# Output weights of the last layer: second half loaded from SyncE's queue, rounding spread over the first block, early minima, scatter waits exchanged

## What is computed

```python
# attention whose mask keeps only keys in the same hash bucket as the query
x = attn_out.transpose(0, 2, 1, 3).reshape(1536, 512)
# mixture of experts, 8 experts, each token goes to one
h = np.maximum(x[mask] @ w1[e], 0.0)
out[mask] = gate_w[mask, None] * eom[mask, e, None] * (h @ w2[e])
# last layer: 1536 x 512 -> 1536 x 2048 -> 1536 x 512
h = x @ w_in
g = np.where(h > 0.0, h, np.exp(np.minimum(h, 0.0)) - 1.0)
return (g @ w_out).astype(np.float32)
```

## Time and profile before

| | |
|---|---|
| median of 3 executions | 815.64 us (815.6 to 816.53) |
| the profiled execution, its own time | 815.6 us |
| its span, first to last instruction | 813.8 us |
| time around the span | 1.8 us |
| mean granted clock of TensorE | 0.999 |
| busy: PE, DVE, ACT, POOL | 97%, 56%, 44%, 42% |
| HBM traffic over the span | 88 GB/s |

### The profile page before, as it was taken

The page is one execution under the profiler, slowest core; times in us unless marked ns, Lnnn a source line. Parts: engine busy times, 40 slices in busy tenths (PEclk is TensorE's granted clock), DMA queues, the critical chain, the costliest instruction groups (busy, mean ns, idle before and its releaser), DMA issues.

```text
span 813.8 us, 12942 instructions
## 1 busy us (share of the span) xinstructions
PE 792.4 (97%) x4389; PEld 658.3 (81%) x4389; DVE 453.5 (56%) x801; ACT 361.6 (44%) x684; POOL 340.4 (42%) x333
## 2 busy tenths in 40 slices
PE   7999999999999889999999999999999999999996
PEld 4777777777777668888888888889889989989985
DVE  5776767777777375454454454549516415613720
ACT  4677676776677413432234330037316405602710
POOL 4334343555556049977797785044210020000000
PEclk9999999999999999999999999999999999999999
DMA  5322232111200047675567660350010020000000
GB/s 151 98 66 76 66 92 94 40 50 42 67 12 18 13 129 277 233 239 199 179 229 236 194 215 18 105 194 0 18 61 2 1 61 17 1 14 27 1 14 26
DMA packets 40942, 72.68 MB, mean 89 GB/s; under 512 B 17904, under 2 KB 24304, under 8 KB 40880
## 3 DMA queue, kind: packets, MB, share of 16 engines
q10 hardware_dynamic: 10608, 33.69, 12.7%
q1 hardware_dynamic: 26832, 26.88, 10.5%
q0 software_dynamic: 3440, 11.28, 4.3%
HBM read 60.56 MB, written 11.28 MB: 88 GB/s over the span
## 4 chain that ended last, share of the span: by engine, by line
PE 92%; DVE 4%; ACT 2%; issue 1%; POOL 1%; DMA 0%; POOLq 0%; ACTq 0%; DVEq 0%
PE pair_t L1350 16%; PE pair_s L1248 13%; PE pair_t L1263 13%; PE pair_u L1118 8%; PE bank_b L1134 8%; PE pair_s L1300 7%; PE pair_u L1300 7%; PE pair_t L1107 4%; PE pair_s L1107 4%; PE bank_b L1145 2%; PE pair_u L1227 2%; PE bank_a L1085 2%; PE bank_a L1093 1%; PE bank_a L1074 1%; DVE g_lo L1054 1%
## 5 line engine op out<-in xcount | busy, mean ns | idle before, releaser
L432 POOL TENSOR_TENSOR w_part<-w_raw,w_part 128x1024 fp32r<-128x1024 f32 x80 | 190.0, 2406 | 51.7 <-ACT w_part L654 51.0
L654 ACT ACTIVATE w_part<-w_raw 128x1024 fp32r<-128x1024 f32 x72 | 73.5, 1055 | 183.8 <-PE pair_t L1263 149.1
L1350 PE MATMUL pair_t<-w_part,g_hi 128*128 128x512 f32 x384 | 118.8, 391 | 0.0
L1248 PE MATMUL pair_s<-w_part,xs_t 128*128 x456 | 108.8, 394 | 0.4 <-DVE xs_t L932 0.4
L1263 PE MATMUL pair_t<-w_part,hid_t 128*128 x456 | 109.0, 394 | 0.0
L563 POOL DMA_INDIRECT out<-o_sb,token x12 | 11.8, 986 | 216.4 <-DVE o_sb L1026 216.4
L1248 PEld LDWEIGHTS pair_s<-w_part,xs_t 128*128 128x128 f32 x456 | 84.2, 188 | 17.8 <-issue 0.9
L1263 PEld LDWEIGHTS pair_t<-w_part,hid_t 128*128 128x128 f32 x456 | 84.4, 189 | 16.8
L1118 PEld LDWEIGHTS pair_u<-first,exps 128*128 128x128 f32 x576 | 65.2, 141 | 27.7 <-ACT exps L614 19.2
L1118 PE MATMUL pair_u<-first,exps 128*128 128x128 f32 x576 | 83.9, 277 | 3.3 <-ACT exps_t L623 1.8
L1350 PEld LDWEIGHTS pair_t<-w_part,g_hi 128*128 128x128 f32 x384 | 71.7, 188 | 14.4
(11 more groups left out here) (196 smaller groups left out, 1214.7 us busy)
## 6 DMA issues: line engine op xcount, KB each, us to landing
w_raw<-in_moe_w ACTq DMA_DIRECT2D x48, 512.0 KB, 6.5
w_raw<-in_moe_w SPq DMA_DIRECT2D x16, 512.0 KB, 8.2
ys_sorted<-ys SPq DMA_DIRECT2D x19, 256.5 KB, 5.7
w_raw<-in_moe_w_in ACTq DMA_DIRECT2D x8, 512.0 KB, 7.1
w_raw<-in_moe_w_out ACTq DMA_DIRECT2D x8, 512.0 KB, 6.6
raw<-in_q SPq DMA_DIRECT2D x16, 192.0 KB, 2.4
raw<-in_k SPq DMA_DIRECT2D x16, 192.0 KB, 2.7
v_nat<-in_v SPq DMA_DIRECT2D x16, 192.0 KB, 2.5
```

Source lines behind the costliest of these rows:

```text
L432: pool.tensor_tensor(chunk_of(w_part, n, 1, c), w_raw[n % 2][c][:, :], chunk_of(w_part, n, 0, c).bitcast(F32), ALU.subtract).then_inc(s_wl ...
L654: act.activation(chunk_of(w_part, n, 0, c), w_raw[n % 2][c][:, :], ACT.Copy).then_inc(s_whi, 1)
L1248: mm = pe.matmul(pair_s[:, h, :], xs_t[:, xp, c * P:(c + 1) * P], w_part[:, bass.ds(par, 1), wp, a:a + 512], start=c == 0 and xp == 0 and ...
L1350: mm = pe.matmul(pair_t[:, t % 2, :], gp[:, f, j * P:(j + 1) * P], w_out_p[:, wp, f, :], start=f == 0 and m == 0, stop=f == FT - 1 and m == 2)
```

## The change

1. Memory: `elu` is placed ahead of `g_lo`, so that it no longer lies over `hid_t`, but over the slots' inputs `xs_raw`.
2. SyncE: before it waits to store the last slot's `ys`, it waits for the end of the last `layer2` and issues the loads of chunks 4 to 7 of w_out.
3. ScalarE: its list of set 9 has only the four loads of the first half. The wait for the last `layer2`, four `w_hi` and four loads in front of the last layer are gone. In block 0 `w_hi` of chunk f // 2 follows every odd step f, from 1 to 15.
4. VectorE: `copy_y(18)` moves from in front of step 0 to in front of step 2 of block 0. The rest of the edit of that loop leaves its order as it was.
5. GpSimd: a scatter waits first for s_o and then for s_tok.

```diff
@@ -240,8 +240,8 @@
             sb("rows_first", [P, BT, YW])
             sb("turned_first", [P, 2, CD, NB], F32R)
             g_hi = sb("g_hi", [P, FT, NB], F32R)
+            elu = sb("elu", [P, 3, NB])
             g_lo = sb("g_lo", [P, FT, NB], F32R)
-            elu = sb("elu", [P, 3, NB])
             o_sb = sb("o_sb", [P, DM])
         w_part = keep("w_part", [P, 2, 2, SET], F32R)
 
@@ -419,6 +419,10 @@
 
 
             for n in range(SLOTS):
+                if n == SLOTS - 1:
+                    wait_release(sp, E + 1, NC1, None)
+                    for c in range(NC1, NCH):
+                        sp.dma_start(chunk_dst(E + 1, c), chunk_source(E + 1, c)).then_inc(s_wld[c], 16)
                 sp.wait_ge(s_y, n + 1)
                 sp.dma_start(ys_dram[n * P:(n + 1) * P, :], ys[:, n % 2, :]).then_inc(s_yst[n % 2], 16)
 
@@ -558,8 +562,8 @@
                                         bass.IndirectOffsetOnAxis(row_at[:, t:t + 1], 0)).then_inc(s_yg[t % BT], 16)
 
             def scatter(t):
+                pool.wait_ge(s_o, t + 1)
                 pool.wait_ge(s_tok, t + 1)
-                pool.wait_ge(s_o, t + 1)
                 pool.indirect_dma_start(out, bass.IndirectOffsetOnAxis(token[:, t:t + 1], 0),
                                         o_sb[:, :], None).then_inc(s_od, 16)
 
@@ -702,7 +706,7 @@
                 if n == 2:
                     ends = load_ends(act, 0, E - 1)
                 if n >= 2:
-                    for c in range(NCH):
+                    for c in range(NCH if n <= E else NC1):
                         if c in (0, NC1):
                             wait_release(act, n, c, ends)
                         if c == NC1:
@@ -734,8 +738,8 @@
                         if blk >= 1:
                             act.wait_ge(s_f2, BT * blk)
                         act.activation(g_hi[:, f - 1, :], elu[:, n % 3, :], ACT.Copy).then_inc(s_gh, 1)
-                        if blk == 0 and f >= NC1 + 2 and f % 2 == 0 and f // 2 + 1 < NCH:
-                            w_hi(E + 1, f // 2 + 1)
+                        if blk == 0 and f % 2 == 1:
+                            w_hi(E + 1, f // 2)
 
 
         @block.vector
@@ -1002,9 +1006,8 @@
             then(dve.tensor_scalar(tile_f[:, :], tile_f[:, :], float(J), float(S - J), ALU.is_ge, ALU.mult))
             then(dve.tensor_tensor(out_row[:, :], part_f[:, :], tile_f[:, :], ALU.add))
 
-            for s in range(SLOTS + 1):
-                if s < SLOTS:
-                    relu(s)
+            for s in range(SLOTS):
+                relu(s)
                 if s + 1 < SLOTS:
                     copy_xt(s + 1)
                 if s == 0:
@@ -1014,8 +1017,7 @@
                     take_yt(0)
                     take_yt(1)
                     take_yt(2)
-                if s < SLOTS:
-                    copy_ht(s)
+                copy_ht(s)
                 if s >= 1:
                     copy_y(s - 1)
 
@@ -1036,6 +1038,8 @@
 
             for blk in range(BLOCKS):
                 for f in range(FT + 2):
+                    if blk == 0 and f == EARLY:
+                        copy_y(SLOTS - 1)
                     if f < FT:
                         n = blk * FT + f
                         dve.wait_ge(s_f1, n + 1)
```

## The result

Nine executions of each kernel: 813.91 us median for the changed one (812.24 to 814.51), 816.41 us for the one before (815.6 to 816.87). The ratio is 0.9969, 95% interval 0.9959 to 0.998, so **faster by 2.5 us**, 0.2 to 0.4%. The forecast was 3.2 us, and 812.4 us with a range up to 813.4. The sign is right. The forecast gain is a quarter too large, and the absolute time lies outside the range.

A forecast was written before the change was run, and what follows sets the result against it. TensorE carries 92% of the chain, so only what leaves it idle can be won. 815.6 - 2.88 (border) - 0.31 (scatter) = 812.4 us, with the seven chunks at 0; range 811.9 to 813.4 us.

The forecast's parts named there:

- The lost 2.88 us at the border: Border between experts and last layer: block 0's 14 hidden tiles take 32.00 us instead of 29.12, all won back.
- the race: Rival: in block 0 GpSimd's reads shut VectorE's low part from the SBUF port; 0.9 us stall, 813.3 us; chance 0.14.
- X: Block 0, from hidden tile 2 to the first output tile: 32.02 us before, forecast 29.12.
- I cost the seven chunks at 0: Block 0: rounding seven w_out chunks and their `w_lo` stall nothing, as VectorE may be 3.0 us late.
- The layout of one step: Block 0: VectorE's next low part starts at m + 3.02, GpSimd at m + 3.11, m being the minimum's start.
- The exchange does nothing: Rival at the kernel's end: exchanging the scatter's two waits gains nothing, time 812.7 us; chance 0.12.
- Covered by 4 us: Block 0's output tiles: the last `w_lo` ends near 575.1, needed at 579.0 and 579.7, so no wait.
- TensorE idle at a chunk of w_out: Sign of being wrong: any idle time of TensorE in block 0 at a chunk of w_out.
- The scatter: Kernel's end: exchanging the last scatter's two waits gives -0.31 us by instruction ends; bounds -0.5 (by starts) and +0.3.
- Gain eaten: Rival: block 0's relevant `w_lo` each cost VectorE 2.12 us; 2.7 us stall, 815.1 us, no change; chance 0.08.
- slower: Rival: block 0, GpSimd's instructions at 2.72 us, always ahead of low part; 4.3 us stall, 816.7 us; chance 0.04.
- Z: From end of last copy to `o_sb` to end of last scatter: 1.74 us before, forecast 1.4.

The follow-up runs named there:

- r7: Kernel before with only the memory placement and VectorE's early minima (`copy_y(18)` moved); 816.49 us against 816.32 for the kernel before.
- r1: The changed kernel run again without an edit; 813.3 us against 815.94 for the kernel before.
- r8: Changed kernel with the loads of chunks 4 to 7 issued by ScalarE behind step 1; 812.7 us against 816.32 for the kernel before.
- r2: Changed kernel with GpSimd's low parts of chunks 1 to 7 halved, each held behind a VectorE low part; 812.18 us against 815.94 before.
- r6: Changed kernel with the scatter's two waits put back as before; 814.04 us against 816.32 for the kernel before.
- r3: Changed kernel with GpSimd setting the low parts of w_out's chunks 1 to 7 to zero; 812.57 us against 815.94 for the kernel before.
- r5: Kernel before with only the scatter's two waits exchanged; 815.81 us against 816.32 for the kernel before.
- r10: Changed kernel with ScalarE's rounding of a chunk ahead of `g_hi`, so GpSimd starts before the low part; 817.96 us against 816.38 before.
- r4: Changed kernel with the copy of the last slot's y back ahead of step 0, so no early minima; 815.18 us against 815.94 before.
- r9: Changed kernel with GpSimd's low parts of chunks 1 to 7 held behind VectorE's, but whole; 812.32 us against 816.38 for the kernel before.

## Why the prediction was wrong in size

**Right.** The lost 2.88 us at the border, and that ScalarE's list ahead of the first exp has to go for any gain (r7). Where the race is not lost in the first two chunks, X is 29.15 (r1, r8; forecast 29.12). Minima 0 and 1 and addition 0 lie before the end of `layer2`, hidden tile 4 does not idle, and the loads on SyncE cost nothing. r2, where the port is out of the way, is 812.18, and its executions with a mean granted clock of 0.999 are 812.03 to 812.18. The sum of 812.4 was thus the sum of a kernel whose port meetings go well. Of the changed kernel's nine executions one, at 812.24, is so short.

**The step that failed** is "I cost the seven chunks at 0". The layout of one step was exact for the first meeting: m + 3.02 against m + 3.11 forecast, 548.47 against 548.57 measured, with m = 545.45. But I carried it to the next meeting with GpSimd's instruction at 2.40 us. It is held too when it arrives in the middle of a low part: 2.71 us. That made the second low part end 0.32 us later than m + 5.93, which used up the idle time before the next minimum and 0.11 us more. My margin was 0.09. I had named the race as a rival with 0.14. It expected 0.9 us of stall among the hidden tiles; measured were 0.60 in X over the forecast, and 0.59 at the output tile, which the rival did not have. Its place in time was wrong. It is not decided once, by chance, but at the second or third chunk, and by a delay that the first meeting brings. Giving a margin of 0.09 us more than four chances to one was the error: of four profiled executions with this order two lost the race at the second chunk (the first, r6) and two at the third (r1, r8).

The Trainium skill ("SBUF — State Buffer", section "Who interferes with whom") states the rule both ways, and says that the second of the two to start blocks fully. I had used one direction only. The trace agrees: held at 548.57, GpSimd's instruction ended 2.26 us after VectorE's low part did, close to its 2.40 us alone. The Trainium skill also says, in the same section, that a VectorE instruction with two SBUF inputs does not contend with a GpSimd instruction that only writes SBUF; r3 shows that, with 0.55 or 0.56 us in all cases.

**"Covered by 4 us"**, the last chunk's low part ahead of the output tile, failed with it. In a chase ScalarE is late with VectorE, and with it the last chunk: it ended at 578.30 + 2.39 = 580.69, with the output tile from 570.79 and wanting it 9.5 us later. That cost 0.59 us, and TensorE idle at a chunk of w_out was a sign of being wrong that I had named. In r1, which lost the race one chunk later, the cover was 0.9 us (579.42 against about 580.3), not 4.

**The scatter** was mis-sized the other way. I took the difference by ends of instructions, 0.31 us, from the first gather. The scatter gives 0.50 in r5 and r6, the bound by starts. That gather's instruction took 1.15 us, 0.2 us longer than the median of its 19, which I read as part of the price.

**The rivals.** "The exchange does nothing" is refuted by r5 and r6. "Gain eaten" and "slower" did not happen, but r10, with GpSimd always ahead, is 1.6 us slower, against 816.7 - 815.6 = 1.1 priced. The wait for `g_hi` has a share in it.

**The range** was set around 815.6 us, one execution and two more. It took no account of the upper group of executions, which the runs shown already had (816.53). That put 0.8 us into the comparison of absolute times. The profiled execution can be added up: 812.4 + 0.85 (start) + 0.60 (X) + 0.59 (output tile) - 0.19 (scatter) = 814.25. Without the late start it would be 813.40, without the lost race 813.06, so the range is left only by both together. Median against median the gain is 2.5 us, and its interval (1.6 to 3.3 us, from the ratio) still reaches to the forecast's 3.2.

**What each part is worth**, by X and Z: ScalarE's list alone 1.0 us (r4: 32.02 to 31.02, with SyncE's loads and one port meeting more), the early minima alone nothing (r7), both together 2.3 to 2.9, the scatter 0.50, SyncE's queue nothing (r8), the rounding spread over the block -1.2 to 0, by how the race falls.

## What to carry to other kernels

When two engines share a port, price the hold in both directions, and follow the pattern over several periods: a margin of a tenth of a microsecond is a tie. Where the order matters, fix it with a semaphore (r9), and if the longer instruction does not fit between two of the other's, cut it (r2); here the semaphore alone gave the same X. And two changes that look like alternatives, an earlier start on one engine and a shorter list on the next, may give nothing and little by themselves, and the whole gain only together.

## What the runs showed of the hardware

- GpSimd's 128x1024 subtraction with two inputs in SBUF takes 2.40 us, and 2.70 to 2.83 when it is the one held by VectorE's 128x384 low part (0.55 us, two inputs in SBUF) that starts within about 0.1 us of it. VectorE's takes up to 2.81 us when it is held. With GpSimd's start recorded 0.01 or 0.02 us ahead it fell either way in executions of one program (the changed kernel and r1).
- Beside GpSimd's 128x1024 memset (0.96 us) the same low part takes its undisturbed 0.55 or 0.56 us (r3).
- A blocked wait directly in front of an indirect DMA, against the same with a passed wait between: 1.74 and 1.75 us against 1.24 or 1.25 us from the end of the copy that releases it to the end of the DMA's instruction.
- TensorE was granted 1.2 GHz for some microseconds early on (0.50 or 0.52 in 16 to 18 us) in seven of the twelve profiled executions, and in r6 and r7 near 300 us instead (0.73 and 0.71 in 298 to 302 us, where before has 1.00). Hidden tile 2 starts at 540.22 to 540.49 us in the three with neither, at 540.89 to 541.66 in the seven, and at 542.02 and 541.70 in r6 and r7. None of the edits changes an engine's list in these stretches. TensorE's busy time in 12 to 14 us does not tell the executions apart: it is 0.60 us in r1, which lost the clock, and 0.40 in r7, which kept it there. What decides it was not tried.
